# Adding scaled expert outputs into the result by accumulating indirect DMAs, with token and weights carried in each row

## What is computed

```python
noisy_logits = x @ w_gate + np.log1p(np.exp(x @ w_noise)) * noise
top2 = np.argpartition(-noisy_logits, 2, axis=1)[:, :2]
top2_w = softmax over the two chosen logits
for e in range(E):
    for k in range(2):
        mask = top2[:, k] == e
        h = np.maximum(x[mask] @ w1[e], 0.0)            # w1[e]: 512 x 1024
        out[mask] += top2_w[mask, k, None] * (h @ w2[e])  # w2[e]: 1024 x 512
```

## Time and profile of the kernel before

| | |
|---|---|
| timed runs | 1189.87 us, median of 3 (1185.16 to 1189.94) |
| the profiled execution's own time | 1201.1 us |
| its span, first to last instruction | 1199.4 us |
| mean granted clock of TensorE | 0.960 |
| PE matmul / weight load | 1088.4 us (91%) / 989.3 us (82%) |
| DVE / ACT / POOL | 514.0 us (43%) / 374.3 us (31%) / 511.5 us (43%) |
| DMA | 156.08 MB, mean 130 GB/s |
| q1 (issued by SP) / q0 (issued by POOL) | 107.40 MB / 48.24 MB |

### The profile page before, as it was taken

The page is one execution under the profiler, slowest core; times in us unless marked ns, Lnnn a source line. Parts: engine busy times, 40 slices in busy tenths (PEclk is TensorE's granted clock), DMA queues, the critical chain, the costliest instruction groups (busy, mean ns, idle before and its releaser), DMA issues. The chain is left out here.

```text
span 1199.4 us, 18749 instructions
## 1 busy us (share of the span) xinstructions
PE 1088.4 (91%) x6340; PEld 989.3 (82%) x6341; DVE 514.0 (43%) x1142; ACT 374.3 (31%) x903; POOL 511.5 (43%) x289
## 2 busy tenths in 40 slices
PE   4999999989999999999993899999999999995770
PEld 4888888867899899999992789898989898984660
DVE  5887778765322333425144422222222232236126
ACT  3777777755222221313131412121212020210100
POOL 7776777720000202012011455555555566657205
PEclk9999999999999999999996799999999999997795
DMA  8644444417599401011011734343443333324218
GB/s 230 146 100 100 98 98 98 98 46 217 194 378 392 170 0 52 5 47 44 9 52 53 269 111 161 130 166 129 149 140 131 140 131 140 131 88 120 81 51 308
DMA packets 83988, 156.08 MB, mean 130 GB/s; under 512 B 9329, under 2 KB 26993, under 8 KB 83953
## 3 DMA queue, kind: packets, MB, share of 16 engines
q1 hardware_dynamic: 70576, 107.40, 29.0%
q0 software_dynamic: 13376, 48.24, 12.0%
HBM read 91.66 MB, written 63.96 MB: 130 GB/s over the span
## 5 line engine op out<-in xcount | busy, mean ns | idle before, releaser
L1396 PE MATMUL ps_hT<-xT_high,ew_high 128*128 128x384 f32 (+1 forms) x512 | 161.5, 315 | 18.4 <-DVE hT_low L1480 14.0
L784 POOL DMA_INDIRECT expert_rows<-x_rows,slot_idx x36 | 37.8, 1049 | 305.9 <-DVE slot_idx L919 296.7
L1396 PE MATMUL ps_hT<-xT_high,ew_low 128*128 128x384 f32 (+1 forms) x512 | 160.2, 313 | 2.2 <-issue 2.2
L1396 PE MATMUL ps_hT<-xT_low,ew_high 128*128 128x384 f32 (+1 forms) x512 | 160.2, 313 | 2.2 <-issue 2.1
L1480 DVE SCALAR_TENSOR_TENSOR hT_low<-ps_hT,hT_high 128x384 fp32r<-128x384 f32 (+1 forms) x128 | 62.3, 490 | 171.1 <-ACT hT_high L1445 153.9
L1411 PE MATMUL ps_y<-ew_high,hT_high 128*128 128x512 f32 x320 | 128.9, 403 | 0.0
L1411 PE MATMUL ps_y<-ew_high,hT_low 128*128 128x512 f32 x320 | 125.6, 392 | 0.0
L1411 PE MATMUL ps_y<-ew_low,hT_high 128*128 128x512 f32 x320 | 124.6, 389 | 0.0
L1396 PEld LDWEIGHTS ps_hT<-xT_high,ew_high 128*128 128x128 f32 x512 | 99.2, 194 | 20.9 <-DVE hT_low L1480 14.2
L1445 ACT ACTIVATE hT_high<-ps_hT 128x384 fp32r<-128x384 f32 (+1 forms) x128 | 55.7, 437 | 193.9 <-PE ps_hT L1396 180.6
L1490 DVE COPY y_tile<-ps_y 128x512 f32<-128x512 f32 x40 | 27.7, 692 | 176.5 <-PE ps_y L1411 176.5
(11 more groups left out here) (213 smaller groups left out, 2725.2 us busy)
## 6 DMA issues: line engine op xcount, KB each, us to landing
spare<-e_w POOLq DMA_DIRECT2D x14, 1024.0 KB, 5.9
w_raw<-e_w POOLq DMA_DIRECT2D x14, 1024.0 KB, 5.5
ex_rows<-expert_rows SPq DMA_DIRECT2D x45, 256.0 KB, 3.9
q_raw<-qT SPq DMA_DIRECT2D x36, 288.0 KB, 4.2
k_raw<-kT SPq DMA_DIRECT2D x36, 288.0 KB, 5.5
expert_rows<-w_raw SPq DMA_DIRECT2D x8, 1280.0 KB, 14.6
expert_out_early<-w_raw SPq DMA_DIRECT2D x8, 1280.0 KB, 14.7
expert_out<-y_tile SPq DMA_DIRECT2D x40, 256.0 KB, 2.3
```

What stands on the lines that cost most here:

```text
L784: nc.gpsimd.indirect_dma_start(out=rows_dram, out_offset=bass.IndirectOffsetOnAxis(ap=slot_idx[:, k, t:t + 1], axis=0), in_=x_rows[:, t, : ...
L1396: mm = nc.tensor.matmul(ps_hT[q % HS][:, 0:rows.stop - rows.start], lhsT[:, c, f * P:(f + 1) * P], rhs[:, c, rows], start=(n == 0), stop=( ...
```

## The change

- **Rows carry more.** A row of `expert_rows` has 516 elements: 512 values, the token number, the weight for the first and for the second expert, and a number that tells the first expert (`idx1`, the expert's index less 100). DVE writes these four columns of `x_rows` before the slots of a group; `slots` and `weights` are gone. Regions are 2560 rows instead of 2304.
- **The output is zeroed** by SP during the routing (12 DMAs over 2944 rows of 512), in place of the unused stretches. `out` has 640 rows more than the result; a slot that holds no row is added there.
- **One loop over stretches** on each engine (`through`): the first and the last stretch are written out, those between are a loop. Weights are loaded and cut for each stretch, by its expert's number. The loads are issued by SP instead of POOL.
- **`know_rows`**, once in each stretch on DVE behind the fifth `low_h`: after it has waited for the loaded rows and the adds of the stretch before, seven instructions on five columns make `out_rows` (the token, or a row behind the result) and `weight_of`.
- **`take_y`** multiplies by `weight_of` as it copies, into five `y_tile` buffers instead of two. **`add_y`**: POOL issues one indirect DMA per tile that adds its 128 rows to `out`.
- `place_outputs`, `order_weights`, the gathers, the mixing and the final stores are gone. The products, their units and their order on PE are the same.
- `plan_experts` makes the first row, the expert, its key and the rows left of each stretch, and the number of stretches less 0 to 3; it has no shifted last stretch.

The diff, cut to its core:

```diff
+            ZEROED = out.shape[0] // P
+            for j in range(0, ZEROED, 2):
+                rows_of = out[j * P:min(j + 2, ZEROED) * P, :].rearrange("(j p) m -> p j m", p=P)
+                sp.dma_start(rows_of, zeros[:, 0:M].unsqueeze(1).to_broadcast([P, min(2, ZEROED - j), M])).then_inc(out_zeroed, 16)
...
+                    dve.wait_ge(e2_ready, g + 1)
+                    link(nc.vector.tensor_scalar(t1["den"][:], t1["e2"][:], 1.0, 1e-9, ALU.add, ALU.add), base)
+                    link(nc.vector.reciprocal(x_rows[:, :, M + 1], t1["den"][:]), base)
+                    link(nc.vector.tensor_tensor(x_rows[:, :, M + 2], t1["e2"][:], x_rows[:, :, M + 1], ALU.mult), base)
+                    link(nc.vector.tensor_copy(x_rows[:, :, M], consts[:, bass.ds(C["token"] + g * TT, TT)]), base)
+                    link(nc.vector.tensor_copy(x_rows[:, :, M + 3], t1["idx1"][:]), base)
...
+        def through(engine, emit):
+
+            _, last, last_but_one, _ = stretches(engine)
+            emit(0, None, False)
+            with engine.Fori(1, last) as g:
+                emit(g, g - 1, False)
+            emit(last, last_but_one, True)
...
+            def cut_high(g, k):
+                loaded, high, _ = piece(k)
+                pool.wait_ge(raw_loaded[k], 16 * g)
+                nc.gpsimd.tensor_tensor(high, loaded, zero.unsqueeze(2).to_broadcast(list(loaded.shape)), ALU.add)\
+                    .then_inc(weights_cut, 1)
+
+            def cut_low(before, k):
+                loaded, high, low = piece(k)
+                pool.wait_ge(weights_cut, 2 * CUTS * before + 2 * k + 1)
+                nc.gpsimd.tensor_tensor(low, loaded, high.bitcast(F32), ALU.subtract).then_inc(weights_cut, 1)
+
+            def add_y(g, j):
+                pool.wait_ge(y_taken, TILES * g + j + 1)
+                pool.sem_inc(waited, 1)
+                nc.gpsimd.indirect_dma_start(out=out, out_offset=bass.IndirectOffsetOnAxis(ap=out_rows[:, j:j + 1], axis=0),
+                                             in_=y_tile[j][:], in_offset=None, compute_op=ALU.add).then_inc(y_added[j], 16)
+
+            def stretch(g, before, last):
+                if before is not None:
+                    pool.wait_ge(y_done, TILES * g)
+                    for k in range(PIECES, 2 * PIECES):
+                        cut_high(g, k)
+                        cut_low(before, k)
+                if last:
+                    for j in range(TILES):
+                        add_y(g, j)
+                    return
+                pool.wait_ge(h_done, UNITS * (g + 1))
+                cut_high(g + 1, 0)
+                cut_low(g, 0)
+                add_y(g, 0)
+                cut_high(g + 1, 1)
+                add_y(g, 1)
+                cut_low(g, 1)
+                for j in range(2, TILES):
+                    add_y(g, j)
...
-            for t in range(T):
-                gather(lower[t], early_dram, 0, t, lower_ready)
-            stored(y_stored, bound(pool, E, E))
-            for t in range(T):
-                if t >= RING:
-                    pool.wait_ge(mixed, t - RING + 1)
-                gather(higher[t % RING][:], out_dram, 1, t, higher_ready[t % RING])
...
+            def next_x(g):
                 sp.wait_ge(x_turned, TILES * g + TILES)
-                sp.sem_inc(waited, 1)
-                load(g + 1)
-                for j in range(TILES):
-                    sp.wait_ge(y_taken, TILES * g + j + 2)
-                    for dst, done in stores:
-                        sp.dma_start(dst[bass.ds(g * STRETCH + j * P, P), :], y_tile[j % YS][:]).then_inc(done[j % YS], 16)
-
-            for s in range(YS):
-                sp.sem_inc(y_stored[s], 16)
-                sp.sem_inc(y_early[s], 16)
-            load(0)
+                sp.wait_ge(rows_known, 2 * (g + 1))
+                load_x(g + 1)
...
-            def take_y(g, j, early):
-                s = j % YS
+            def know_rows(g, first):
+
+                for j in range(TILES):
+                    dve.wait_ge(x_loaded[j], 16 * (g + 1))
+                    if not first:
+                        dve.wait_ge(y_added[j], 16 * g)
+                left, key = rows_left[:, bass.ds(g, 1)], expert_key[:, bass.ds(g, 1)]
+                place = consts[:, C["place"]:C["place"] + TILES]
+                nc.vector.tensor_scalar(is_held[:], place, left, None, ALU.is_lt).then_inc(rows_read, 1)
+                nc.vector.tensor_scalar(is_first[:], x_rows[:, :, M + 3], key, None, ALU.is_equal).then_inc(rows_read, 1)
+                nc.vector.tensor_copy(token_of[:], x_rows[:, :, M]).then_inc(rows_read, 1)
+                nc.vector.tensor_copy(out_rows[:], nowhere[:]).then_inc(rows_read, 1)
+                nc.vector.tensor_copy(weight_of[:], x_rows[:, :, M + 2]).then_inc(rows_read, 1)
+                dve.wait_ge(rows_read, READS * (g + 1))
+                dve.sem_inc(waited, 1)
+                nc.vector.copy_predicated(out_rows[:], is_held[:], token_of[:]).then_inc(rows_known, 1)
+                nc.vector.copy_predicated(weight_of[:], is_first[:], x_rows[:, :, M + 1]).then_inc(rows_known, 1)
+
+            def take_y(g, j):
                 dve.wait_ge(y_done, TILES * g + j + 1)
-
-                dve.wait_ge(y_stored[s], 16 * (g * len(range(s, TILES, YS)) + j // YS + 1))
-                if early:
-                    dve.wait_ge(y_early[s], 16 * (g * len(range(s, TILES, YS)) + j // YS + 1))
-                nc.vector.tensor_copy(y_tile[s][:], ps_y[s][:]).then_inc(y_taken, 1)
-
-            def stretch(g, early):
+                if j == 0:
+                    dve.wait_ge(rows_known, 2 * (g + 1))
+                nc.vector.tensor_scalar(y_tile[j][:], ps_y[j % YS][:], weight_of[:, j:j + 1], None, ALU.mult).then_inc(y_taken, 1)
+
+            def stretch(g, before, last):
                 for q in range(UNITS):
                     low_h(g, q)
+                    if q == FC // 2:
+                        know_rows(g, before is None)
...
-            place_outputs(nc, dve, place_step, rows_placed, consts, C, plan, slots, out_rows_i, room)
-            for s in range(YS):
-                dve.wait_ge(y_early[s], 16 * (begin * len(range(s, TILES, YS)) + 1))
-                dve.sem_inc(waited, 1)
-            with dve.Fori(begin, total) as g:
-                stretch(g, False)
-
-            order_weights(nc, dve, weights_step, slot_weights, weights, room)
-            dve.wait_ge(lower_ready, 16 * T)
-            for t in range(T):
-                r = t % RING
-                nc.vector.tensor_scalar(lower[t], lower[t], weights[:, 0, t:t + 1], None, ALU.mult).then_inc(scaled, 1)
-                dve.wait_ge(higher_ready[r], 16 * (t // RING + 1))
-                dve.wait_ge(scaled, t + 1)
-                nc.vector.scalar_tensor_tensor(out=lower[t], in0=higher[r][:], scalar=weights[:, 1, t:t + 1], in1=lower[t],
-                                               op0=ALU.mult, op1=ALU.add).then_inc(mixed, 1)
...
```

More of the change, by code:

```diff
@@ L665, in gated_product_and_routing @@
     w1_high, w1_low, w2_high, w2_low, wo_high, wo_low = parts
-    rows_dram, outs_dram, slots, weights, counts = store
+    rows_dram, out, counts = store
     DC, N = xT.shape[1], xT.shape[2]
@@ L1105, in plan_experts @@
-    link(nc.vector.tensor_reduce(bounds, each(E + 1, E), AX.X, ALU.add))
-    link(nc.vector.tensor_copy(bounds_i[:], bounds))
-    link(nc.vector.tensor_scalar(unused[:], stretches[:], -float(STRETCH), float(REGION), ALU.mult, ALU.add))
-    link(nc.vector.tensor_scalar(held, held, float(STRETCH), None, ALU.max))
-    link(nc.vector.scalar_tensor_tensor(out=shift[:], in0=stretches[:], scalar=float(STRETCH), in1=held,
-                                        op0=ALU.mult, op1=ALU.subtract))
+    link(nc.vector.tensor_tensor(each(E, K), along(held, K), across(limits, E), ALU.is_gt))
@@ new lines, in plan_experts @@
+    link(nc.vector.tensor_reduce(stretches, each(E, K), AX.X, ALU.add))
+    link(nc.vector.tensor_scalar(stretches, stretches, 1.0, None, ALU.max))
+    link(nc.vector.tensor_tensor(each(E + 1, E), earlier, across(stretches, E + 1), ALU.mult))
+    link(nc.vector.tensor_reduce(bounds, each(E + 1, E), AX.X, ALU.add))
+    for k in range(ends_i.shape[1]):
+        link(nc.vector.tensor_scalar(ends_i[:, k:k + 1], bounds[:, E:E + 1], -float(k), None, ALU.add))
+    add_up(number, bounds[:, 1:E], ones, ALU.is_ge, expert_of)
@@ L1360, in _, with next_second, next_first @@
+            def next_second(g, before):
+                e = expert(g + 1)
+                for k in range(PIECES, 2 * PIECES):
+                    sp.wait_ge(weights_cut, 2 * CUTS * before + 2 * (k + 1))
+                    load_w(e, k)
+            def next_first(g):
+                e = expert(g + 2)
+                for k in range(PIECES):
+                    sp.wait_ge(weights_cut, 2 * CUTS * g + 2 * (k + 1))
+                    load_w(e, k)
+            load_x(0)
             for k in range(PIECES, 2 * PIECES):
@@ L1371, in _ @@
```

(27 more changed lines are left out.)

319 lines of the change are left out of this document (111 added, 208 removed).

## The result

The changed kernel takes **1219.2 us** (median of 4 runs, 1219.1 to 1222.2) against 1189.9 before: 1.026 times as long [1.0228, 1.0292]. The forecast was 1187, its range 1138 to 1207, and "slower" had a chance of 0.25. The profiled execution took 1222.2 us, its span is 1220.2.

The account below looks back on a forecast made before the run. PE was taken to bound the expert stage, with losses in the eighth stretch and the tail. 1201.1 - 30.3 - 31.6 + 1.0 + 52.5 = 1192.7, less 5.6 carried over, gave 1187 us; range 1138 to 1207.

Parts of the forecast that it names:

- the hold-up: In seven stretches, POOL's cuts hold `know_rows` on DVE, so PE waits 5.9 us each; with low clock, +52.5 us.
- the rival of one pause: All five reads of `know_rows` pass in one pause between POOL's cuts; PE waits 1.0 per stretch: 1142 us, chance 0.26.
- the one without a hold-up: Rival: the new `know_rows` instructions are not held by POOL's cuts, leaving only gains: 1134.6 us, chance 0.12.
- The rival of indirect transfers that disturb PE: Each of 40 adds makes PE pause and lowers its clock, 20 to 33 us more: 1207 to 1220, chance 0.15.
- the routing: Five linked DVE instructions ahead of the slot numbers cost +1.0 us once, on the last group; slack covers the others.
- the low clock behind the rests: After each wait of 5.9 us PE runs at half pace, losing 1.6 us per stretch (bounds 0 to 1.6).
- the tail: Behind the last y_tile only one indirect add is left, its landing taken as 3.0 us: -31.6 us (-29 to -32.3).
- The carry-over to the runs: Half of the 11.2 us by which the profiled execution exceeded the median is subtracted: -5.6 us.
- the eighth stretch: Without `place_outputs` and the gathers it falls back from 88.1 to the others' 57.8 us: -30.3 us.

Follow-up runs that it names:

- know_late: The changed kernel with `know_rows` moved from behind the fifth `low_h` to behind the thirteenth: 1162.3 us, 0.9766 of the kernel before.
- before_mis32: The kernel before with only 32 unused bytes per partition put behind `ex_rows`: 1194.1 us, 1.003 of the kernel before.
- before_64: The kernel before with only 64 unused bytes per partition put behind `ex_rows`: 1190.8 us, 1.0006 of the kernel before.
- meta_early: The changed kernel with the routing's five linked DVE instructions moved from ahead of the slot numbers to f == 5: 1212.8 us, 1.019 of the kernel before.
- all_regs: The changed kernel with `know_rows` late, extra columns written early, 96 unused bytes behind `ex_rows`, and two plan numbers loaded per engine, PE's ahead of `turn_x`: 1141.0 us.
- plain_scatter: The changed kernel with rows stored at their places instead of added, so the two results are not summed: 1214.5 us in one execution.
- all_at0: all_regs with 32 unused bytes behind `ex_rows` instead of 96: 1150.7 us, 0.9673 of the kernel before.
- aligned: The changed kernel with 96 unused bytes per partition put behind `ex_rows`: 1213.6 us, 1.0197 of the kernel before.

## Why the prediction was wrong

**The mechanism of the hold-up was right.** A rest of 5.9 us was forecast for each of seven stretches, because one or two instructions pass between two cuts; 6.0 was measured, know_late took it away, and the rival of one pause (1142) and the one without a hold-up (1134.6) both fall. The count inside is different from `place_outputs`: two reads held, then three instructions close together (the last starts 0.01 us behind the start of POOL's fourth cut, so the rows don't tell whether a COPY is held at all), and a predicated copy held. The Trainium skill, VectorE: DVE Perf Modes, section Mode 2×_2P, has odd outermost dimensions take both port pairs when source and destination are equal; the trace agrees, with 2.4 and 3.2 us on average for two five-column TENSOR_SCALARs that take 0.23 alone. The rival of indirect transfers that disturb PE fell as well: beside 40 adds no wait of PE's matmuls names "issue". That its price, 1207 to 1220, holds the measured 1219.2 is luck.

**Four terms were off**, each to the slow side: the routing, for which the slack was read from the wrong group, the pace, the low clock behind the rests, and the tail. Against the own time of the profiled execution, 1192.7 were forecast and 1222.2 came, 29.5 more:

- *The routing*, +1.0 forecast. The first first product starts at 682.56 instead of 670.65, 11.9 later: **10.9** more. Of the 11.9, 2.6 lie ahead of the routing (its first copy to x_rows starts at 354.41 instead of 351.82), in code that the change leaves alone; in before_mis32 and before_64 that copy starts at 354.10 and 353.81, so this part is a difference between executions and not the change. Another 6.2 come in from group to group, 1.3 to 1.7 in each of four steps and nothing in the last. The sentence that failed is that "1.7 us of slack cover the 1.0, and also a scatter of rows that are 16 bytes longer". Rows 9 and 10 are of the last group, where the loop's code is written out once more and PE comes later. In the loop the slack was 0.1 us once and 1.2 three times (rows above, under meta_early). And the delay was larger than 1.0: in three of the groups the scatter starts 1.25 us later and its six DMAs take 9.0 us for 7.8, so ACT's copy is released 2.5 to 2.8 us later. meta_early takes away the first of these and keeps the second, which then just fits into the slack; why the six DMAs take longer, no run here shows. The last 3.1 us lie behind the groups: 1.7 until PE turns the first loaded rows, where 1.0 was forecast, and 1.4 from there to the first product, in which register loads behind the turning, which I did not count, lengthen PE's pause by 1.6 (all_regs).
- *PE's pace*, nothing forecast. 0.93 us in each of eight stretches: **7.4**. I took "the products, their units and their order on PE are the same" for the same time. That 516 instead of 512 numbers in a row move the operands in SBUF didn't occur to me, and no row of before shows what that costs. The sentence isn't quite true either: PE no longer turns rows behind the last stretch, which makes that one 1.9 us shorter (56.83 for 58.73 in know_late).
- *The stretches' rests and clock.* From the first product to the end of the last one 529.4 us passed; before it was 492.1, and with 30.3 taken off and 52.5 added 514.3 were forecast. Of the **15.1** more, 7.4 are the pace above, less the 1.9; 0.8 are the rests (42.1 for 41.3); 1.7 are a longer first stretch, beside its pace, with a mean clock of 0.96 for 0.98; 1.1 were never there to be taken off, since the 88.1 us of the earlier trace rows begin 0.2 us ahead of the first product and end 0.9 behind the last. What is left, **6.0**, is clock behind the seven rests: each of these stretches is 7.7 to 9.0 us longer than its counterpart in know_late, 6.0 of it the rest. 1.6 us for each was forecast, by the window behind the 14.0 us wait, and 2.5 came. The rests are shorter than 14.0 us, but the low clock behind some of them lasts longer: 3.1 to 6.0 us, for 3.7 behind the long one (the 3.3 read from the earlier trace rows stop at the end of their window).
- *The tail.* From the end of the last product to the own time of the execution 10.2 us pass (1222.2 less 1211.95), for 6.8 forecast: **3.5**. Behind the last y_tile, which is ready at 1212.74, POOL starts 0.8 us later instead of at once; the add lands 4.7 us after that start, for the 4.2 of an issue and a landing added up (the landings in the DMA view are counted from the start of the issue, so the issue is in them); and 1.9 us more pass until the last instruction of the program, for which the forecast had nothing. The other 0.3 lie around the span. I had leaned on the plain store for the landing. 2.0 of the tail are the addition's: behind the last y_tile 7.4 us remain with it and 5.4 in plain_scatter.

10.9 + 15.1 + 3.5 = 29.5.

**The carry-over to the runs.** I subtracted 5.6 us as half of what the profiled execution of before had above its median; that of after had 3.0. The "issue" pauses of 8.6 us were that one execution's: in before_mis32 and before_64, the same kernel but for unused bytes, no wait of PE names "issue" at this place, and the eighth stretch, from its first product to its second, takes 44.5 and 44.2 us for the 28.1 to 28.2 of others. So at the median the eighth stretch was worth some 16 us and not 30.3. In the same two executions the experts began 2.0 and 2.9 us later than in the one that I read, which is why the whole was only 11.2 above its median. An estimate with these: 1189.9 - 16 - 31.6 + 1.0 + 52.5 = 1195.8, so even at the median some 23 us were missing.

The misses lay outside my bounds: a clock term of 0 to 1.6 us a stretch, -29 to -32.3 for the tail, and no bounds at all for the routing and the pace. The range took in an error of the hold-up, and none of the terms set to about nothing.

## What to carry to other kernels

Ask of each small SBUF-to-SBUF instruction that a change adds on DVE whether POOL is cutting then: seven 0.2 us instructions cost 57 us of 1219 in one place and nothing eight units later. Read the slack in every group of a loop, not only in the iteration that is written out by itself. And when a change alters the sizes of tiles, compare PE's time for the same group of matmuls before and after: 96 unused bytes gave back 1.5 us in each stretch here.

## What was not expected

- The place of operands in SBUF changes the time of the same stretch by up to 2.6% (57.25 to 58.74 us), with rows that show PE busy throughout. It is repeatable from kernel to kernel; within one, a single stretch of all_at0 is 0.1 us shorter than its neighbours.
- A COPY_PREDICATED of five columns is held by a cut of POOL like a TENSOR_SCALAR: 3.72 us on average instead of 0.17.
- Behind the seven rests of 6 us the clock stays at 0.50 for 3.1 to 6.0 us; after the 14.0 us wait of before it was 3.7 us.
- An indirect DMA that adds takes POOL 1.56 us and lands in 4.9; without the addition 0.97 and 2.7.
- A faster PE waits longer: in the run aligned, of the time won in pace 4.8 us went into the wait for the same cuts.
- The version with all four edits, all_regs, takes 1141.0 us, 0.9584 of the kernel before. The idea of the change is good for 50 us. Of the 78 us between the change as made and this version, 57 are the place of seven small instructions.
